# Attention, mixture of experts and gated feed-forward in one kernel: the softmax divisor is moved into the attention loop, and the stage behind attention is written anew

## The reference

```python
def _attn_ref(q, k, v, s):            # [4, 8, 576, 64], s [4, 8, 576]
    scores = scale * np.matmul(q, k.transpose(0, 1, 3, 2))
    cum = np.cumsum(np.maximum(s, 0.0), axis=-1)
    bias = -(cum[:, :, :, None] - cum[:, :, None, :])
    scores = np.where(causal, -1000000000.0, scores + np.minimum(bias, 0.0))
    scores = scores - np.max(scores, axis=-1, keepdims=True)
    attn = np.exp(scores)
    attn = attn / (np.sum(attn, axis=-1, keepdims=True) + 1e-09)
    return np.matmul(attn, v)
def _moe_ref(x, w_gate, w_noise, noise, w1, w2):      # 8 experts, 512 -> 1024 -> 512
    noisy_logits = x @ w_gate + np.log1p(np.exp(x @ w_noise)) * noise
    # the two largest of 8 per token; weights by softmax over the two
    ...
            h = np.maximum(x[mask] @ w1[e], 0.0)
            out[mask] += top2_w[mask, k, None] * (h @ w2[e])
def _moe2_ref(x, w_gate, w_val, w_out):               # 512 -> 1536 -> 512
    return (1.0 / (1.0 + np.exp(-(x @ w_gate))) * (x @ w_val)) @ w_out
```

## Time and profile before

| what | us |
|---|---|
| median of 3 runs | 1274.19 (1273.27 to 1275.47) |
| the profiled execution, whole | 1277.16 |
| its span in the trace | 1275.4 |
| PE, DVE, ACT, POOL busy | 1237.4, 497.1, 512.6, 361.6 |
| granted TensorE clock, mean | 0.987 of full speed |

### The profile page before, as it was taken

One profiled execution on the slowest core, in us unless ns is written; L12 is line 12 of the kernel. 1 busy time (PEld: TensorE's weight loads), 2 busy tenths in 40 slices (PEclk: granted clock), 3 DMA queues, 4 the chain that ended last, 5 costly groups with the idle time before them and its releaser, 6 DMA issues.

```text
span 1275.4 us, 23476 instructions
## 1 busy us (share of the span) xinstructions
PE 1237.4 (97%) x7362; PEld 1073.5 (84%) x7363; DVE 497.1 (39%) x924; ACT 512.6 (40%) x1184; POOL 361.6 (28%) x410
## 2 busy tenths in 40 slices
PE   8999999779999999999999999899999999999998
PEld 7777877478888888888888888799999999999997
DVE  7788886825060606050505080522231221313211
ACT  5888887743334343333433333412122121221211
POOL 4224541024443545453444463301010100100000
PEclk9999999689999999999999999999999999999999
DMA  4723232343242664233332411302010100100000
GB/s 101 203 62 77 65 69 78 108 134 100 65 148 82 214 199 146 92 122 105 109 124 90 148 33 42 116 2 71 4 51 25 42 34 0 49 25 0 25 1 25
DMA packets 100414, 101.57 MB, mean 80 GB/s; under 512 B 70196, under 2 KB 70196, under 8 KB 100336
## 3 DMA queue, kind: packets, MB, share of 16 engines
q1 hardware_dynamic: 82832, 64.06, 17.0%
q0 software_dynamic: 7280, 20.86, 5.9%
q10 hardware_dynamic: 10256, 16.06, 3.6%
HBM read 80.05 MB, written 22.73 MB: 81 GB/s over the span
## 4 chain that ended last, share of the span: by engine, by line
PE 86%; DVE 6%; issue 3%; ACT 3%; DMA 1%; DVEq 0%; ACTq 0%; POOL 0%; POOLq 0%
PE PB L1591 10%; PE PB L1590 10%; PE PB L1589 10%; PE PD L1589 9%; PE PD L1591 9%; PE PD L1590 9%; PE PA L1591 4%; PE PA L1589 4%; PE PA L1590 4%; PE PC L1440 3%; PE PC L1624 3%; ACT xtok L913 2%; DVE probT L1069 2%; PE PB L1486 2%; DVE Q L1059 2%
## 5 line engine op out<-in xcount | busy, mean ns | idle before, releaser
L1287 DVE CAST WX<-raw 128x1024 fp32r<-128x1024 f32 x56 | 56.4, 1007 | 278.0 <-DMA raw<-in_moe_w 278.0
L1330 DVE TENSOR_TENSOR gv<-sig,PB 128x384 f32<-128x384 f32 x72 | 39.9, 555 | 296.5 <-PE PB L1591 286.9
L757 POOL TENSOR_TENSOR hsTl<-hsT,hsTh 128x512 fp32r<-128x512 f32 x84 | 122.2, 1476 | 113.7 <-ACT hsT L968 113.7
L1589 PE MATMUL PB<-WX,xsTh 128*128 x344 | 138.0, 401 | 1.8 <-POOL xsTl L748 1.8
L1591 PE MATMUL PB<-WX,xsTl 128*128 x344 | 135.5, 394 | 0.0
L1589 PE MATMUL PD<-WX,hsTh 128*128 x336 | 135.2, 402 | 0.2 <-issue 0.2
L1590 PE MATMUL PB<-WX,xsTh 128*128 x344 | 135.3, 393 | 0.0
L1591 PE MATMUL PD<-WX,hsTl 128*128 x336 | 131.6, 392 | 0.0
L1590 PE MATMUL PD<-WX,hsTh 128*128 x336 | 130.9, 390 | 0.0
L1006 ACT ACTIVATE sig<-PA 128x384 f32<-128x384 f32 x72 | 35.4, 492 | 184.4 <-PE PA L1591 184.4
L1011 ACT ACTIVATE gvh<-gv 128x384 fp32r<-128x384 f32 x72 | 37.8, 525 | 160.2 <-DVE gv L1330 160.2
(11 more groups left out here) (246 smaller groups left out, 2664.9 us busy)
## 6 DMA issues: line engine op xcount, KB each, us to landing
raw<-in_moe_w SPq DMA_DIRECT2D x28, 1024.0 KB, 5.2
y_d<-ys ACTq DMA_DIRECT2D x43, 256.0 KB
out<-fin SPq DMA_DIRECT2D x18, 256.0 KB, 2.1
qin<-in_q SPq DMA_DIRECT2D x32, 128.0 KB, 2.4
vin<-in_v SPq DMA_DIRECT2D x32, 128.0 KB, 2.4
raw<-in_moe_w ACTq DMA_DIRECT2D x4, 1024.0 KB
x_d<-xtok SPq DMA_DIRECT2D x16, 256.0 KB, 2.0
kin<-in_k SPq DMA_DIRECT2D x28, 128.0 KB, 2.4
```

Source lines behind the costliest of these rows:

```text
L757: nc.gpsimd.tensor_tensor(hsTl[:, cols], hsT[:, cols], hsTh[:, cols].bitcast(F32), ALU.subtract).then_inc(hTl_done, 1)
L1287: nc.vector.tensor_copy(high, source).then_inc(w_high, 1)
L1330: nc.vector.tensor_tensor(gv[:, :], sig[:, :], PB[:, 512 * (f % 2):512 * (f % 2) + GN], ALU.mult).then_inc(gv_done, 1)
L1589: pe.matmul(acc, hi, w_hi, start=first, stop=False)
```

## The change

**1/sum goes into the attention loop.** ACT adds 1e-9 to a pair's sums (`r_added`), DVE takes the reciprocal, PE turns the [128, 10] result to [10, 128] (`turn_r`), ACT copies it to `r_rows` (`r_copy`), SP stores it to DRAM `r_d` (`store_r`) and loads each head's row back spread over 64 partitions into `RT` (`load_r`). DVE multiplies the pair's output with `RT` while it moves it to `xT` (`out_scaled`) in the next odd step; ACT's `copy_out` is gone. The last pair's spread is made by POOL (`r_wide`) and five transposes. **The drain is reordered.** The gate products need no division; a gate's sum is one reduction over 4 chunks. x leaves PSUM undivided, two tiles per ACT instruction of 1024 columns: 12 groups and 12 stores instead of 20 tiles. **The one-hots** become wide comparisons of 16-bit tiles with the 20 tiles innermost; `ROUND` finds the block by rounding. `BUSY` is (8, 16, 5).

```diff
-BUSY = (8, 28, 12)
+BUSY = (8, 16, 5)
...
+                def r_added():
+                    pr = 2 * g_ + (u - 4) // 2
...
+                    nc.scalar.activation(r_sum[u // 2][:, :, :], rs[:, 2 * pr:2 * pr + 2, :] if isinstance(pr, int) else
+                                         rs[:, bass.ds(2 * pr, 2), :], ACT.Copy, bias=1e-9).then_inc(r_summed, 1)
...
+                    nc.scalar.activation(r_rows[0:2 * QT, :], PA[0:2 * QT, KPAD:KPAD + P], ACT.Copy).then_inc(r_copied, 1)
...
+                    pe.wait_ge(r_ready, pr + 1)
+                    pe.sem_inc(pe_passed, 1)
+                    pe.transpose(PA[0:2 * QT, KPAD:KPAD + P],
+                                 rinv[u // 2][:, :, :].rearrange("p h j -> p (h j)"), ident[:, :]
+                                 ).then_inc(r_turned, 1)
...
+            def load_r(pr):
+
+                sp.wait_ge(out_copied, pr + 1)
+                sp.sem_inc(sp_passed, 1)
+                sp.wait_ge(r_stored, 16 * (pr + 1))
+                sp.sem_inc(sp_passed, 1)
+                for u in range(2):
+                    row = r_d[2 * pr + u:2 * pr + u + 1, 0:S] if isinstance(pr, int) else r_d[bass.ds(2 * pr + u, 1), 0:S]
+                    sp.dma_start(RT[D * u:D * u + D, :], row.to_broadcast([D, S])).then_inc(r_loaded, 16)
...
+                    dve.wait_ge(weighted, pair + 2)
+                    if last:
+                        dve.wait_ge(last_r_copied, 1)
+                    else:
+                        dve.wait_ge(r_loaded, 32 * (pair + 1))
...
+                                            PD[:, 0:S], RT_last if last else RT[:, :], ALU.mult
+                                            ).then_inc(out_copied, 1)
...
+                if j1 < QT:
+                    nc.scalar.activation(xtok[n % XB][:, :, :].rearrange("p j d -> p (j d)"), bank[:, :], ACT.Copy
+                                         ).then_inc(x_copied, 1)
...
+        X_GROUPS = [(b, j0, j1) for b in range(B) for j0, j1 in ((0, 2), (2, 4), (4, 5))]
...
+            dve.wait_ge(rconst, 5)
             for n in range(2):
+                nc.vector.tensor_tensor(ohhi[n][:, :, :], block16[:, :, :], over_b(block_of[:, n, :]), ALU.is_equal
+                                        ).then_inc(blocks_made, 1)
+                if n == 0:
+                    nc.vector.tensor_tensor(ohlo[n][:, :, :], slot16[:, :, :],
+                                            slot_of[:, n, :].unsqueeze(1).to_broadcast([P, P, TT]), ALU.is_equal
+                                            ).then_inc(slots_ready, 1)
```

More of the change, by code:

```diff
@@ L932, in _ @@
+            attention(act, one_step)
+            act.wait_ge(last_r_turned, 1)
+            nc.scalar.activation(RT_last, PA[:, 0:S], ACT.Copy).then_inc(last_r_copied, 1)
+            for b in range(B - 1):
+                gate_copy(b)
+            act.wait_ge(out_copied, PAIRS + 1)
+            gate_copy(B - 1)
+            act.wait_ge(g_summed, B)
+            act.wait_ge(rconst, 2)
             nc.scalar.activation(spl[:, :, :], glog[:, :, E:2 * E], ACT.Abs).then_inc(act_step, 1)
@@ L1104, in one_step @@
                             low(x, 1)
+                elif isinstance(hp, int) and hp == HEADS - 1:
+                    reciprocals()
+                    out_scaled()
+                    copy(3)
+                    copy(4)
                 elif u % 2 == 0:
@@ L1121, in one_step @@
                     least(3)
+                    if not (isinstance(g_, int) and 4 * g_ + u > HEADS + 1):
+                        out_scaled()
                     low(0)
@@ L1550, in behind, with turn_x @@
[L1550 to L1566 removed]
+            def turn_x(n):
+                b, j0, j1 = X_GROUPS[n]
+                bank = (PB, PC)[n % 2]
+                if n == 0:
+                    pe.wait_ge(masked, HEADS * QT)
+                elif n == 1:
+                    pe.wait_ge(g_summed, B)
+                else:
+                    pe.wait_ge(x_copied, n - 1)
+                for j in range(j0, j1):
+                    for c_ in range(DC):
+                        at = 512 * (j - j0) + P * c_
+                        last = pe.transpose(bank[0:ROWS[j], at:at + P], xT[:, DC * b + c_, P * j:P * j + ROWS[j]],
+                                            ident[:, :])
+                last.then_inc(x_turned, 1)
+                if n:
+                    keep_busy(1, PA)
@@ L1569, in _ @@
+            attention(pe, one_step)
+            gate_rows(0)
+            for b in range(1, B):
+                gate_turned(b)
+            for b in range(1, B):
+                gate_rows(b)
+            for n in range(6):
+                turn_x(n)
             pe.wait_ge(ohs_ready, 1)
-            pe.wait_ge(rconst, 3)
-            flat = ohs[:, :, :].rearrange("p e t -> p (e t)")
+            pe.wait_ge(rconst, 2)
+            flat = ohs[:, :, :].rearrange("p t e -> p e t")
             pe.matmul(PD[:, 512:512 + E * TT], ones[:, :], flat, start=True, stop=True).then_inc(counted, 1)
```

468 lines of the change are left out of this document (255 added, 213 removed).

## The result

The changed kernel took 1268.94 us, median of five runs (1265.17 to 1269.72); the kernel before, on the same chip, 1274.45 (1273.27 to 1276.35). The ratio is 0.9948, 95% interval [0.9933, 0.9963]: faster by 5.5 us where 14.4 had been forecast, and 0.9 above the range's upper end of 1268.0.

The account below looks back on a forecast made before the run. PE bounds attention and the experts; the drain's chain to the gather delays the whole. +1.4 (attention) - 14.3 (gather) - 1.5 (first block) = -14.4 from 1277.16, 1262.8; less 2.97 to the median: 1259.8 us, range 1253.5 to 1268.

Parts of the forecast that it names:

- Attention: Attention loop: DVE's multiplication sticks out about 0.1 us a pair, the other additions hidden; +1.4 us over 14 pairs.
- rival 4: Attention's odd step: DVE waits for `RT`, each pair losing about 1.3 us; 1279 us, slower than before; chance 4%.
- The pair: A pair of heads in attention: 12.88 us before, about 0.1 more from DVE, ACT's two small instructions at nothing.
- Up to the softplus: Drain, from the last value product to softplus: softplus starts at 231.9 us instead of 234.12.
- Routing and one-hots: Drain after softplus: scan at 238.6 us instead of 243.13, one-hots from 242.4 instead of 247.93, taking 7.3.
- The list's end: After DVE's one-hots: PE's last ten products 0.4 us, `idx` 0.3, 0.84 to the gather at 251.2.
- The pitch of 40 bytes: One-hots read as PE's weights: twenty products 2.7 us instead of 0.67, second half about 1 us later, 1261.
- x: Drain's x copies and stores: 12 copies, 4.72 MB stored in 13.3 us, gather not before 250.4 us.
- rival 2: Drain: stores at 213 GB/s take 22.2 us, gather at 259.3, +8.1 us; 1268 us, chance 8%.
- rival 1: Drain: TensorE at half clock through the x groups, gather near 257, +6 us; 1266 us, chance 15%.
- rival 3: Attention: DVE becomes the bound, additions cost 13.8 us instead of 1.4; 1272 us, chance 7%.
- First block: Idle products behind the gather's arrival fall from 24 instructions to 10, -2.5 us, clock takes 1.0 back: -1.5 us.

Follow-up runs that it names:

- runs 1 to 3: On the changed kernel: first expert's 4 MB issued by SP behind the `RT` load, 1261.46 us; ten side loads behind `RT`, 1267.07; both, 1258.95.
- runs 11 to 13: On e3_both: `xT` copy back on ACT, 1258.81 us; DVE's multiplication behind the low part, 1269.75; reciprocals turned twice, 1260.16; ACT's reciprocal copy last, 1259.11.
- f2_contig: e3_both with the slot one-hots and their constant laid with the 128 slots innermost, so PE's weights adjoin: 1262.90 us.
- run 8: e3_both with the block one-hots laid with the 43 blocks innermost, weights at their old pitch: 1260.83 us.
- e3_both: Changed kernel with the first expert's 4 MB moved behind the `RT` load and ten side loads behind `RT`: 1258.95 us; on another chip 1261.85.
- e2_side: Changed kernel with the ten router and noise loads behind the `RT` load of pair 11 and the v load: 1267.07 us.
- e4_rt_first: Changed kernel with the `RT` load ahead of the six q and k issues for pair 0 alone, 4 MB left in place: 1263.60 us.
- f1_xb6: e3_both with six x buffers instead of four: 1259.87 us.
- f4_busy: e3_both with `BUSY` back to (8, 28, 12), the idle products of before around the gather: 1266.78 us.
- h2_busy28: e3_both with `BUSY` (8, 28, 5), 28 idle products ahead of the gather's arrival instead of 16: 1264.89 us.
- g4_busy12: e3_both with `BUSY` (8, 16, 12), twelve idle products behind the gather's arrival instead of five: 1261.86 us.

## Why the prediction was wrong

The direction was right and the size was not: 5.5 us measured for 14.4, outside the range.

- **The step that failed** is the one on SP in "Attention", which let every load of `RT` land in time and so put this wait at nothing: "SP gets three transfers a pair and two waits. Behind them are the next q, k and v loads, which have about a pair's time to spare. `RT` is needed one pair after its rows are copied". The mechanism that I priced as rival 4 did occur, but not in every pair: it took one landing of 13 us and one issue 6 us late. I had worked out the landing from the drain's 2.23 us and from attention's mean DMA share of 0.33; for nearly all of the 30 loads that holds (median 3.0 us). The trace of before had the exception in plain sight: its window 36 to 48 us has a DMA share of 1.00, and ACT's four 1 MB issues stand in it. Likewise I counted the six q and k issues ahead of `RT` and not the ten side loads, which stand at the one place where the loop over pairs is written out. I also took the rival to be slower than before or nothing. The runs showed in place of that step two waits of DVE, 4.94 and 1.42 us, and with what PE lost to the half clock and to ACT's issues runs 1 to 3 put the two meetings at 8.4 us together by the traces.
- **The pair.** 0.1 us was forecast for DVE, 0.13 came (13.01 against 12.88), but from ACT: "I cost both together at nothing" was wrong for the second instruction, and the multiplication sticks out by nothing (runs 11 to 13).
- **Up to the softplus.** From the last value product's end to softplus 6.1 us instead of 7.1, forecast 6.5. Together with the pair this is right to 0.5 us once the two waits are gone.
- **Routing and one-hots.** Softplus to scan 7.07 us (forecast 6.7), scan to one-hots 4.02 (3.8), one-hots 5.15 (7.3, lower bound 5.1). The middle was too careful: instructions with all operands of 16 bits do run at twice the rate (2560 elements in 1.48 us, 860 in 0.61 where rows 11 have 1.06). The 0.6 us that the sum took for the fixed parts of seven instructions does not follow from its own slope, which gives 0.157 each, 1.1; successive rows overlap by some 0.09 us, which is why 0.6 came near. The Trainium skill ("VectorE: DVE Perf Modes", "The perf-mode tier table") had it; 2560 elements in 1.48 us here and 2.81 with 32-bit inputs agree. The Trainium skill ("Advanced Engine Details and Errata", "Mode Summary") asks for unit stride besides; f2_contig agrees, where an operand whose innermost stride is 0 costs the whole gain.
- **The list's end.** `idx` starts 1.6 us behind DVE's last comparison (257.94, 259.57), where I had 0.4, and the gather 1.5 behind that instead of 1.1. The pitch of 40 bytes, which the forecast named as a possible microsecond, is real: forty products take 3.48 us instead of 1.34 (two times 0.67), but the moving operand's pitch does it as well as the weights' (run 8), and the factor is 2.6 and not 4.1. So it is luck that the gather stands at the forecast distance from softplus; the errors cancel: +0.4, +0.2, -2.15, +1.2 and +0.4 make 0.1.
- **x** ended with the list, as forecast, but not ahead of it: the last store is issued at 257.60 us, takes 2.5 to land and is there at 260.1, and `idx` is done at 259.77. In the changed kernel POOL was released by the store, by 0.3 us; in e3_both by the list. From the first store's issue (243.79) to the last landing are 16.3 us, where 15.5 were forecast and 24.4 would have been rival 2, which is false. TensorE's clock is 1.00 in 234 to 256 us (rival 1 false), and DVE did not bind (rival 3 false).
- **First block.** From the gather to the first block's `hs` copy 11.6 us instead of 13.9: -2.3 for a forecast of -1.5. The 1.0 us that I expected the clock to take back did not come in this block: the clock is 1.00 in 264 to 274 us, where it had been 0.83 before. Behind the block another 0.8 us are gained that the forecast had not (gather to end 1006.8 us, 1009.9 before); what gave them is open.

## What to carry to other kernels

A transfer's landing is not a price per kind but per place: before a load is given a deadline, look at the DMA share of the stretch in which each of its instances falls, the first ones above all, and not at the mean of the loop. In a queue that issues in order, the first and last turns that are written out by hand hold other things than the loop. Where two things end together, look at the landing and not at the issue: x was handed over 1.7 us earlier and landed no earlier. And a small instruction put ahead of what another engine waits for costs time (0.13 us a pair for a copy of 0.25), however much its own engine idles elsewhere; at the end of the step it was free in four pairs of five.

## What the runs showed of the hardware

- 4 MB in flight from one queue delayed a 288 KB load that was issued 3 us later on another by 10 us (13.0 in the changed kernel and 13.7 in e2_side, median 3.0). In e4_rt_first, where the load went out just ahead of them, it landed in 7.9 us.
- Issuing itself became slower in the same stretch: SP's two k issues took 5.05 us (e4_rt_first) and 1.15 in e3_both, ACT's last two of the 4 MB 2.58 us (e4_rt_first) and 1.17 in the kernel before.
- A store issued 1.75 us earlier landed no earlier: 4.4 us from issue to landing in f1_xb6, 2.5 in e3_both.
- PE's 16-bit products with operands at a pitch of 40 bytes: 1.45 us for twenty when it is the weights, 1.75 when it is the 43 moving columns, 1.89 when it is both, 0.67 when neither.
- DVE's double rate on 16-bit data is lost if one operand's innermost stride is 0 (f2_contig: 2.82 us for 2560 elements) and kept if an operand is spread on a middle axis (1.48 us).
- A wait of PE of 2.25 and 1.93 us on nothing that the profile shows stood some 770 us behind twelve more idle products, in both of the kernels on e3_both that had them (f4_busy, h2_busy28); seven more behind the gather did not bring it (g4_busy12), and the kernel before, with as many as f4_busy, has none. Its cause is open.
